# Local attention cut into ten windows of 64 keys, in place of nine windows of 72

## The chip, the cores and the metric

The kernel runs on one core of a Trainium2 chip, in one launch. The metric is the device time in microseconds (us) of that core, from one execution. The engines are TensorE (PE in the profile, with its weight loads as PEld), VectorE (DVE), ScalarE (ACT), GpSimd (POOL) and SyncE (SP), which issues nearly all of the DMAs.

## What is computed

Two kinds of attention on 2 batches of 8 heads of 576 tokens with 64 dimensions, whose outputs are added; then two feed-forward layers on the 1152 tokens of width 512. The change touches only the local attention.

```python
q_d = q.reshape(B, H, S // 4, 4, D).mean(axis=3)      # the same for k_d, v_d
out_up = np.repeat(sm_attn(q_d, k_d, v_d), 4, axis=2)
mask = np.abs(pos[:, None] - pos[None, :]) < 4
scores = np.where(mask, scale * q @ k.T, -1e9)
out_local = softmax(scores) @ v
x = out_up + out_local                                # heads side by side: 1152 x 512
h = x @ w_in;  g = np.where(h > 0, h, exp(min(h, 0)) - 1);  x = g @ w_out
# then four experts: sum_e p_e * relu(x @ w1[e]) @ w2[e], with 1024 hidden columns each
```

A query sees itself and three tokens on each side, so a chunk of n queries needs n + 6 keys.

## The kernel before

Heads are taken in pairs, eight pairs in all (`PAIRS`); a pair's two heads sit in partitions 0 to 63 and 64 to 127. The pairs 0 to 3 (batch 0) are worked on one after the other at the head of the kernel (mode ALONE, some 40 us). The pairs 4 to 7 (batch 1) are spread over the four blocks of the first feed-forward layer of batch 0 (mode MIXED): one pair to a block of 16 groups of matmuls (`mixed_block1`, L576). After that nothing of the attention is left, and the rest of the first layer and the four experts follow. The matmuls of the feed-forward layers are done in three products of a high and a low part (`product` L521, `product2` L593).

One pair takes these steps. `turn_q` and `turn_k` (L402, L411) bring q and k to 64 x 576 per head by transposes on TensorE. `score` (L425) has three parts j: j = 0 is the pooled attention, j = 1 and 2 are the local one, in chunks 0 to 3 and 4 to 8 of 64 queries (`SPANS` L39), each against a window of 72 keys (`WIN`). For the local parts a bf16 matmul of an identity and a band of 0 and -1e9 first writes the mask into the PSUM bank (L449), then the scores are added to it (L456). Both heads have matmuls of their own: head 0 on rows and columns 0 to 63 of the array, head 1 on rows and columns 64 to 127. Then DVE takes the row maxima of a part (`row_max` L1210), ACT the exponentials with their sums, chunk by chunk (`exponentiate` L867, line L877), DVE the reciprocals (L1221), and POOL multiplies (`normalise` L1620, line L1623). `turn_attn` (L461) transposes each chunk of 128 x 72 on its own; the last chunk, 8, has a place of its own in PSUM (`last_at` L99, line L487), the others four to a bank (L491). ACT copies them to SBUF (`copy_attnT` L882, lines L886 and L889). `mix` (L495) multiplies with v: first the pooled part (L510), then chunk by chunk and head by head (L516), 72 keys deep, head 0 into columns 0 to 63 and head 1 into columns 64 to 127. ACT copies the pooled result (L895), DVE adds both (`add_outputs` L1238, line L1246), and the sum is split into a high part (ACT L901) and a low one (DVE L1253).

In the trace an f32 matmul stands as two records of PE (two passes), each with its weight load; a transpose and the bf16 or fp32r matmuls are one record each.

All orders are written out by hand, engine by engine: for PE L780 to L848, for ACT L1089 to L1150, for POOL L1701 to L1728. In a mixed block (L576) the scores stand behind group 3, the three `turn_attn` behind groups 8, 10 and 11, and `mix` behind group 13. A group g waits until the bank of group g - 4 is free (`bank_free1` L529), which for g from 4 to 11 means that DVE has written its low part (`elu_lo` L1263, line L1266). ACT has the exponentials of the three parts in groups 4, 6 and 8, and the copies in 10 and 12 (L1135).

`load_v` (L320) loads the windows of v by four DMAs for a pair: for each head one with chunks 1 to 7 (L326) and one with chunks 0 and 8 (L329). SP issues, in this order, q of pair 0, q and k of pair 1, v of 0, q and k of 2, v of 1, q and k of 3, v of 2 and 3, q and k of 4, and only then the first weights `wa_raw` (L361) and `wb_raw` (L362). ACT turns the first weights into their high part (`first_wa` L1084, line L1087) at a fixed place in its order, between steps of pairs 1 to 3 (L1117).

## Time and profile before

| what | value |
|---|---|
| median of 3 runs | 647.47 us (647.23 to 647.62) |
| profiled execution, its own time | 647.4 us |
| its span in the trace | 645.6 us |
| PE busy | 638.2 us (99%), 4743 records |
| DVE, ACT, POOL busy | 349.4, 285.8, 323.2 us |
| granted TensorE clock | full over the whole span |
| DMA | 46.13 MB, mean 71 GB/s |

The busy time of an engine is the time in which at least one of its instructions is under way. A matmul of 64 columns stands in the trace with some 220 ns from its start to its end, and several are under way at once, so that the share of 99% says that PE seldom waits long; how dense the matmuls stand is read from their starts.

### The profile page before, as it was taken

To read this page: it belongs to the slowest core of one execution; us is meant where nothing else is said; L and a number is where in the kernel's file an instruction comes from. 1 tells how busy PE (TensorE), PEld (TensorE's weight loads), DVE (VectorE), ACT (ScalarE), POOL (GpSimd) and SP (SyncE) were. 2 spreads that over 40 slices of the span, in tenths; PEclk is the share of its full clock that TensorE was granted. 3 is DMA by queue.
4 is the path that set the end of the run, shared out by engine and by line. 5 is a ranking of instruction groups with operands and counts; after the bars stand their busy time and mean duration, and the time that the engine had idled before them with its cause. 6 is when DMAs were issued, how large, how long until landed. Compare 5 with 4: busy or idle time off the path is not lost.

```text
span 645.6 us, 13042 instructions
## 1 busy us (share of the span) xinstructions
PE 638.2 (99%) x4743; PEld 592.7 (92%) x4743; DVE 349.4 (54%) x764; ACT 285.8 (44%) x778; POOL 323.2 (50%) x278
## 2 busy tenths in 40 slices
PE   8999999999999999999999999999999999999998
PEld 5889999999999999998899899899899899889986
DVE  5976454545557787764453464355365255365352
ACT  4887474747476676553142152052152142142210
POOL 3684435353397999888238047056065164160200
PEclk9999999999999999999999999999999999999999
DMA  9963615142123223203003011011011012020012
GB/s 191 213 185 92 142 67 141 65 105 65 66 71 126 65 66 117 79 0 132 1 22 111 1 56 74 0 65 65 0 65 65 0 65 65 1 66 2 0 50 97
DMA packets 51491, 46.13 MB, mean 71 GB/s; under 512 B 31616, under 2 KB 33920, under 8 KB 51456
## 3 DMA queue, kind: packets, MB, share of 16 engines
q1 hardware_dynamic: 50272, 45.38, 23.9%
q10 hardware_dynamic: 1184, 0.30, 0.2%
q8 instruction: 21, 0.34, 0.2%
q14 instruction: 14, 0.11, 0.1%
HBM read 43.30 MB, written 2.36 MB: 71 GB/s over the span
## 4 chain that ended last, share of the span: by engine, by line
PE 94%; DVE 2%; ACT 1%; DMA 1%; issue 1%; POOL 0%; SPq 0%; DVEq 0%
PE psum L524 16%; PE psum L526 16%; PE psum L525 16%; PE psum L596 11%; PE psum L600 11%; PE psum L598 11%; PE psum L666 2%; PE psum L665 2%; PE psum L664 2%; PE psum L456 1%; PE psum L442 1%; PE psum L516 1%; PE psum L491 1%; PE psum L471 1%; DMA q_in<-in_q 1%; PE psum L570 1%
## 5 line engine op out<-in xcount | busy, mean ns | idle before, releaser
L1628 POOL TENSOR_TENSOR wb_lo<-wb_raw,wb_hi 128x512 fp32r<-128x512 f32 x64 | 81.8, 1298 | 183.3 <-ACT wb_hi L911 183.3
L1438 DVE SCALAR_TENSOR_TENSOR o_acc<-psum,gate_now,o_acc 128x512 f32<-128x512 f32 x72 | 54.0, 750 | 126.0 <-PE psum L526 125.7
L526 PE MATMUL psum<-wb_hi,h_lo 128*128 128x512 f32 x288 | 112.3, 390 | 0.0
L525 PE MATMUL psum<-wb_lo,h_hi 128*128 128x512 f32 x288 | 112.2, 390 | 0.0
L524 PE MATMUL psum<-wb_hi,h_hi 128*128 128x512 f32 x288 | 112.0, 389 | 0.0
L1021 ACT ACTIVATE h_hi<-psum 128x320 fp32r<-128x320 f32 (+1 forms) x128 | 52.5, 412 | 87.3 <-DVE psum L1410 40.3
L1628 POOL TENSOR_TENSOR wa_lo<-wa_raw,wa_hi 128x512 fp32r<-128x512 f32 x60 | 77.6, 1318 | 16.8 <-ACT wa_hi L952 16.8
L1027 ACT COPY sums<-psum 128x256 f32<-128x256 f32 (+1 forms) x32 | 12.8, 400 | 155.1 <-PE psum L600 155.1
L600 PE MATMUL psum<-x_hi,wa_lo 128*128 128x256 f32 (+2 forms) x228 | 67.4, 296 | 0.0
L598 PE MATMUL psum<-x_lo,wa_hi 128*128 128x256 f32 (+2 forms) x228 | 67.3, 295 | 0.0
L596 PE MATMUL psum<-x_hi,wa_hi 128*128 128x256 f32 (+2 forms) x228 | 67.2, 295 | 0.0
L526 PEld LDWEIGHTS psum<-wb_hi,h_lo 128*128 128x128 f32 x288 | 54.1, 188 | 11.3
L1392 DVE SCALAR_TENSOR_TENSOR h_lo<-psum,h_hi 128x320 fp32r<-128x320 f32 (+1 forms) x128 | 54.8, 450 | 17.1 <-ACT h_hi L1021 17.0
L525 PEld LDWEIGHTS psum<-wb_lo,h_hi 128*128 128x128 f32 x288 | 54.1, 188 | 10.9
L524 PEld LDWEIGHTS psum<-wb_hi,h_hi 128*128 128x128 f32 x288 | 54.1, 188 | 10.8
L524 PE MATMUL psum<-h_hi,wb_hi 128*128 128x288 f32 x160 | 48.9, 306 | 0.0
L526 PE MATMUL psum<-h_hi,wb_lo 128*128 128x288 f32 x160 | 47.1, 294 | 0.0
L525 PE MATMUL psum<-h_lo,wb_hi 128*128 128x288 f32 x160 | 47.1, 294 | 0.0
L598 PE MATMUL psum<-t_lo,s_hi 128*128 128x320 f32 (+2 forms) x152 | 44.9, 295 | 0.0
L600 PE MATMUL psum<-t_hi,s_lo 128*128 128x320 f32 (+2 forms) x152 | 44.8, 295 | 0.0
L596 PE MATMUL psum<-t_hi,s_hi 128*128 128x320 f32 (+2 forms) x152 | 44.8, 295 | 0.0
L596 PEld LDWEIGHTS psum<-x_hi,wa_hi 128*128 128x128 f32 x228 | 43.0, 189 | 0.6
(195 smaller groups left out, 1684.2 us busy)
## 6 DMA issues: line engine op xcount, KB each, us to landing
wa_raw<-in_moe_w_in SPq DMA_DIRECT2D x8, 1024.0 KB, 5.5
wb_raw<-in_moe_w_out SPq DMA_DIRECT2D x8, 1024.0 KB, 5.1
wa_raw<-in_moe_w SPq DMA_DIRECT2D x8, 1024.0 KB, 4.9
wb_raw<-in_moe_w SPq DMA_DIRECT2D x8, 1024.0 KB, 5.0
out<-o_acc SPq DMA_DIRECT2D x9, 256.0 KB, 2.0
q_in<-in_q SPq DMA_DIRECT2D x10, 144.0 KB, 3.9
v_in<-in_v SPq DMA_DIRECT2D x5, 288.0 KB
v_win<-in_v SPq DMA_DIRECT2D x10, 126.0 KB
```

Of the source, the lines that this page charges most:

```text
L524: nc.tensor.matmul(bank_cols, w_hi(n), x_hi_(n), start=(n == 0), stop=False)
L525: nc.tensor.matmul(bank_cols, w_hi(n), x_lo_(n), start=False, stop=False)
L526: last = nc.tensor.matmul(bank_cols, w_lo(n), x_hi_(n), start=False, stop=(n == chunks - 1))
L596: nc.tensor.matmul(bank, w_op[0][:, k, :], x_op[0][:, k, :], start=(start and k == 0), stop=False, skip_group_check=True)
L598: nc.tensor.matmul(bank, w_op[0][:, k, :], x_op[1][:, k, :], start=False, stop=False, skip_group_check=True)
L600: last = nc.tensor.matmul(bank, w_op[1][:, k, :], x_op[0][:, k, :], start=False, stop=(stop and k == 1), skip_group_check=True)
L664: nc.tensor.matmul(to, wb_hi[:, f, cols], h_hi[:, f, t], start=(f == 0), stop=False)
L665: nc.tensor.matmul(to, wb_hi[:, f, cols], h_lo[:, f, t], start=False, stop=False)
L1021: nc.scalar.activation(h_hi[:, 2 * fh + p, t0 + width * th:t0 + width * (th + 1)], psum[:, bank[p], 0:width], ACT.Relu).then_inc(h_hi_read ...
L1392: nc.vector.scalar_tensor_tensor(h_lo[at], bank(banks, p), 0.0, h_hi[at].bitcast(F32), ALU.max, ALU.subtract).then_inc(h_lo_ready, 1)
L1438: nc.vector.scalar_tensor_tensor(o_acc[:, m, :], psum[:, DOWN2_BANKS[(MT * half + m) % 2], :], gate_now[:, m:m + 1], o_acc[:, m, :], ALU.m ...
L1628: nc.gpsimd.tensor_tensor(lo[:, c, :], raw[:, c, :], hi[:, c, :].bitcast(F32), ALU.subtract).then_inc(lo_ready, 1)
```

## The change

The local attention is cut into ten chunks (slots) of at most 58 queries with windows of 64 keys, in place of nine of 64 queries and 72 keys. Even slots are the first half of the tokens and odd slots the second half (`TOK_AT`). A slot's scores are still computed for 64 queries (`Q_AT`), and only its own 58 (56 in the last two) are used by `mix`.

Slots 0 to 3 are part j = 1, slots 4 to 9 part j = 2. In part 2 the heads change places: head 0 writes to PSUM partitions 64 to 127 and head 1 to 0 to 63 (`part_of`). In the mixed blocks `local_scores` writes both masks and then issues the scores of the two parts by turns, so that four neighbouring matmuls lie in the four 64 x 64 corners of the array, and the two parts in two banks. In mode ALONE the parts stay apart.

`turn_attn` turns two slots (128 x 128) by one transpose, five in place of nine, with an even slot's keys in partitions 0 to 63 and an odd slot's in 64 to 127. The last chunk's own place, its waits and its copy are gone: `copy_attnT` makes two copies (128 x 256 and 128 x 384) in place of three. `v_win` has the windows of the even slots in partitions 0 to 63 and those of the odd slots in 64 to 127; it is loaded by eight DMAs in place of four. `mix` has 20 matmuls, 64 keys deep with 58 moving columns, in place of 18 of 72 keys with 64 columns, and goes round the four corners; the even slots' results go to one bank and the odd slots' to the other, in place of chunks 0 to 3 and 4 to 8. The exponentials are ten of 64 columns in place of nine of 72. In the lines left out, `OUT_SPLIT` becomes 288, the buffers and `band_of` follow the new shapes, `mixed_block1` calls `local_scores(u)` in place of parts 1 and 2 of `score`, PE's wait for `attnT_copied` ahead of `turn_q(3)` goes, and `copy_attnT_p` counts three transpose signals to a pair.

```diff
@@ -27,9 +27,14 @@
-NQT = SEQ // QT
-WIN = QT + 2 * FACTOR
-WIN_START = [min(max(QT * c - FACTOR, 0), SEQ - WIN) for c in range(NQT)]
+WIN = 64
+QSTEP = WIN - 2 * (FACTOR - 1)
+CHUNKS = -(-HALF // QSTEP)
+NQT = 2 * CHUNKS
+TOK_AT = [HALF * (s % 2) + QSTEP * (s // 2) for s in range(NQT)]
+TOK_N = [min(QSTEP, HALF - QSTEP * (s // 2)) for s in range(NQT)]
+Q_AT = [min(t, SEQ - QT) for t in TOK_AT]
+WIN_AT = [min(max(t - FACTOR + 1, 0), SEQ - WIN) for t in TOK_AT]
...
@@ -37,9 +42,8 @@
-LAST = NQT - 1
-BAND_RUNS = (None, ((0, 1), (1, 4)), ((4, LAST), (LAST, NQT)))
-BAND_PAD = QT * LAST - WIN_START[LAST]
+BAND_RUNS = (None, ((0, 1), (1, 4)), ((4, NQT - 1), (NQT - 1, NQT)))
+BAND_PAD = FACTOR - 1
...
@@ -96,11 +100,9 @@
-def last_at(u, mode):
-    if mode == MIXED:
-        return 0, 0
-    return (1, HALF) if u == HALF_PAIRS - 1 else (7, HALF)
+def part_of(h, j):
+    return slice(QT * h, QT * (h + 1)) if j < 2 else slice(QT * (1 - h), QT * (2 - h))
...
@@ -156,10 +158,10 @@
-                    spare[0:WIN, win_at:win_at + NQT * 2 * HD].rearrange("p (c h d) -> p c h d", h=2, d=HD))
+                    spare[:, win_at:win_at + CHUNKS * 2 * HD].rearrange("p (c h d) -> p c h d", h=2, d=HD))
         own_set = (sb1("q_in", [LT, NLT, 2 * HD])[:], sb1("k_in", [LT, NLT, 2 * HD])[:],
-                   sb1("v_in", [PT, 4, FACTOR * HD])[:], sb1("v_win", [WIN, NQT, 2, HD])[:])
+                   sb1("v_in", [PT, 4, FACTOR * HD])[:], sb1("v_win", [2 * WIN, CHUNKS, 2, HD])[:])
...
@@ -320,15 +322,17 @@
-                for h in range(2):
-                    at = rows.offset + h * SEQ * HD
-                    sp.dma_start(win[:, 1:NQT - 1, h, :],
-                                 bass.AP(rows.tensor, at + WIN_START[1] * HD,
-                                         [[HD, WIN], [QT * HD, NQT - 2], [1, HD]])).then_inc(win_loaded[held(u)], 16)
-                    sp.dma_start(win[:, 0:NQT:NQT - 1, h, :],
-                                 bass.AP(rows.tensor, at,
-                                         [[HD, WIN], [WIN_START[-1] * HD, 2], [1, HD]])).then_inc(win_loaded[held(u)], 16)
+                for e, (i0, odd) in enumerate(((1, 0), (0, CHUNKS - 1))):
+                    part = slice(WIN * e, WIN * (e + 1))
+                    for h in range(2):
+                        at = rows.offset + h * SEQ * HD
+                        sp.dma_start(win[part, i0:i0 + CHUNKS - 1, h, :],
+                                     bass.AP(rows.tensor, at + WIN_AT[2 * i0 + e] * HD,
+                                             [[HD, WIN], [QSTEP * HD, CHUNKS - 1], [1, HD]])).then_inc(win_loaded[held(u)], 16)
+                        sp.dma_start(win[part, odd, h, :],
+                                     bass.AP(rows.tensor, at + WIN_AT[2 * odd + e] * HD, [[HD, WIN], [1, HD]])
+                                     ).then_inc(win_loaded[held(u)], 16)
...
@@ -422,6 +426,27 @@
+            def band_masks(j, bank):
+                c0 = SPANS[j][0]
+                for n, (e0, e1) in enumerate(BAND_RUNS[j]):
+                    for h in range(2):
+                        rows = slice(HD * h, HD * (h + 1))
+                        nc.tensor.matmul(psum[part_of(h, j), bank, WIN * (e0 - c0):WIN * (e1 - c0)],
+                                         ident2[rows, rows], band_of(h, e0, e1), start=(n == 0), stop=False,
+                                         skip_group_check=True)
+            def local_score(u, j, s, bank):
+                at = WIN * (s - SPANS[j][0])
+                for h in range(2):
+                    rows = slice(HD * h, HD * (h + 1))
+                    last = nc.tensor.matmul(psum[part_of(h, j), bank, at:at + WIN],
+                                            qT[slot(u)][rows, Q_AT[s]:Q_AT[s] + QT], kT[slot(u)][rows, WIN_AT[s]:WIN_AT[s] + WIN],
+                                            start=False, stop=(s == SPANS[j][1] - 1), skip_group_check=True)
+                if s == SPANS[j][1] - 1:
+                    last.then_inc(scored, 1)
...
@@ -441,22 +466,22 @@
+                    last.then_inc(scored, 1)
                 else:
-                    c0, c1 = SPANS[j]
-                    for n, (e0, e1) in enumerate(BAND_RUNS[j]):
-                        for h in range(2):
-                            rows = slice(HD * h, HD * (h + 1))
-                            nc.tensor.matmul(psum[QT * h:QT * (h + 1), bank, WIN * (e0 - c0):WIN * (e1 - c0)],
-                                             ident2[rows, rows], band_of(h, e0, e1), start=(n == 0), stop=False,
-                                             skip_group_check=True)
-                    for c in range(c0, c1):
-                        s = WIN_START[c]
-                        for h in range(2):
-                            rows = slice(HD * h, HD * (h + 1))
-                            last = nc.tensor.matmul(psum[QT * h:QT * (h + 1), bank, WIN * (c - c0):WIN * (c - c0 + 1)],
-                                                    qT[slot(u)][rows, QT * c:QT * (c + 1)], kT[slot(u)][rows, s:s + WIN],
-                                                    start=False, stop=(c == c1 - 1), skip_group_check=True)
-                last.then_inc(scored, 1)
+                    band_masks(j, bank)
+                    for s in range(*SPANS[j]):
+                        local_score(u, j, s, bank)
+            def local_scores(u):
+                banks = [score_bank(u, j, MIXED) for j in range(3)]
+                band_masks(1, banks[1])
+                band_masks(2, banks[2])
+                first, second = range(*SPANS[1]), range(*SPANS[2])
+                for n in range(len(second)):
+                    if n < len(first):
+                        local_score(u, 1, first[n], banks[1])
+                    local_score(u, 2, second[n], banks[2])
...
@@ -474,22 +499,10 @@
-                if j == 2:
-                    if mode == MIXED:
-                        pe.wait_ge(attnT_p_copied, 2 * u + 1)
-                    elif u < 2:
-                        pe.wait_ge(qT_copied, u + 3)
-                    elif u == 2:
-                        pe.wait_ge(out_free, 2 * u + OUT_CREDIT)
-                    else:
-                        pe.wait_ge(qT_copied, HALF_PAIRS + 1)
-                    bank, at = last_at(u, mode)
-                    nc.tensor.transpose(psum[0:WIN, bank, at:at + 128], attn[:, LAST, :], ident[:]
-                                        ).then_inc(attn_turned, 1)
-                c0, c1 = SPANS[j]
-                for c in range(c0, min(c1, LAST)):
-                    last = nc.tensor.transpose(psum[0:WIN, TURN_BANKS[mode][j], 128 * (c - c0):128 * (c - c0 + 1)],
-                                               attn[:, c, :], ident[:])
+                for i in range(SPANS[j][0] // 2, SPANS[j][1] // 2):
+                    at = 128 * (i - SPANS[j][0] // 2)
+                    last = nc.tensor.transpose(psum[:, TURN_BANKS[mode][j], at:at + 128],
+                                               attn[:, 2 * i:2 * i + 2, :].rearrange("p e k -> p (e k)"), ident[:])
...
@@ -500,22 +513,23 @@
-                pe.wait_ge(win_loaded[held(u)], 64 * loads(u))
+                pe.wait_ge(win_loaded[held(u)], 128 * loads(u))
                 pe.wait_ge(attnT_p_copied, 2 * u + 2)
-                pe.wait_ge(attnT_copied, 3 * u + 3)
+                pe.wait_ge(attnT_copied, 2 * u + 2)
                 for kc in range(2):
                     for h in range(2):
                         nc.tensor.matmul(psum[HD * h:HD * (h + 1), banks[0], OUT_SPLIT:OUT_SPLIT + POOLED],
                                          v_sum[slot(u)][:, 2 * h + kc, :], attnT_p[slot(u)][:, kc, h, :], start=(kc == 0), stop=(kc == 1))
-                for half in range(2):
-                    c0, c1 = SPANS[half + 1]
-                    for c in range(c0, c1):
-                        for h in range(2):
-                            last = nc.tensor.matmul(psum[HD * h:HD * (h + 1), banks[half], QT * (c - c0):QT * (c - c0 + 1)],
-                                                    v_win[held(u)][:, c, h, :], attnT[:, c, QT * h:QT * (h + 1)],
-                                                    start=True, stop=True)
+                for i in range(CHUNKS):
+                    for e, h in ((0, 0), (1, 1), (0, 1), (1, 0)):
+                        c = 2 * i + e
+                        rows = slice(WIN * e, WIN * (e + 1))
+                        q0 = part_of(h, 1 if c < SPANS[1][1] else 2).start + TOK_AT[c] - Q_AT[c]
+                        last = nc.tensor.matmul(psum[HD * h:HD * (h + 1), banks[e], QSTEP * i:QSTEP * i + TOK_N[c]],
+                                                v_win[held(u)][rows, i, h, :], attnT[rows, i, q0:q0 + TOK_N[c]],
+                                                start=True, stop=True)
...
@@ -869,7 +881,7 @@
-                    act.wait_ge(attn_turned, 4 * (u - 1) + (1, 2, 4)[j])
+                    act.wait_ge(attn_turned, 3 * (u - 1) + j + 1)
...
@@ -880,14 +892,9 @@
-                if j == 2:
-                    act.wait_ge(attn_turned, 4 * u + 3)
-                    bank, at = last_at(u, mode)
-                    nc.scalar.copy(attnT[:, LAST, :], psum[0:WIN, bank, at:at + 128]).then_inc(attnT_copied, 1)
-                c0, c1 = SPANS[j][0], min(SPANS[j][1], LAST)
-                act.wait_ge(attn_turned, 4 * u + 2 * j)
-                nc.scalar.copy(attnT[:, c0:c1, :], psum[0:WIN, TURN_BANKS[mode][j], 0:128 * (c1 - c0)]
-                               ).then_inc(attnT_copied, 1)
+                i0, i1 = SPANS[j][0] // 2, SPANS[j][1] // 2
+                act.wait_ge(attn_turned, 3 * u + j + 1)
+                nc.scalar.copy(attnT[:, i0:i1, :], psum[:, TURN_BANKS[mode][j], 0:128 * (i1 - i0)]).then_inc(attnT_copied, 1)
...
```

## Rows read from the trace of the kernel before

**Rows 1.** The page: busy us, share of the span, and instructions of each engine.

```profile
PE 638.2 (99%) x4743; PEld 592.7 (92%) x4743; DVE 349.4 (54%) x764; ACT 285.8 (44%) x778; POOL 323.2 (50%) x278
```

**Rows 2.** Busy us by stretch: length, PE, PEld, DVE, ACT, POOL, clock, DMA share, GB/s.

```profile
5.00:40.30 35.30, 32.68 (x533) 27.82 (x533) 29.26 (x69) 28.93 (x123) 21.91 (x27) 1.00 0.94 213
...
46.00:167.00 121.00, 121.00 (x1202) 118.46 (x1202) 63.35 (x160) 73.58 (x239) 56.96 (x53) 1.00 0.37 100
...
22.00:34.00 12.00, 11.45 (x203) 9.74 (x203) 11.77 (x28) 10.29 (x49) 10.64 (x15) 1.00 0.97 246
```

**Rows 3.** Groups by line and shape, PE: busy us, mean ns of one | idle.

```profile
L491 PE MATMUL psum<-ident,attn 128*72 128x128 f32 x64 | 9.6, 273 | 0.0
...
L516 PE MATMUL psum<-attnT,v_win 72*64 72x64 f32 x180 | 6.1, 222 | 0.0
```

**Rows 4.** Timeline of PE, scores of the second mixed block: start us, us from first start to last end.

```profile
78.88 0.95 PE L442 MATMUL psum<-kTs,qTs 64*64 64x144 f32 x12
79.67 0.29 PE L449 MATMUL psum<-band,ident 64*64 64x72 bf16 x4
79.80 0.67 PE L456 MATMUL psum<-kT,qT 64*64 64x72 f32 x16
80.30 0.32 PE L449 MATMUL psum<-band,ident 64*64 64x288 bf16 x4
80.45 0.82 PE L456 MATMUL psum<-kT,qT 64*64 64x72 f32 x20
81.20 0.40 PE L524 MATMUL psum<-x_hi,wa_hi 128*128 128x288 f32 x1
```

**Rows 5.** Timeline of PE, two narrow windows at the first two records of L442.

```profile
46.12 0.33 PE L442 MATMUL psum<-kTs,qTs 64*64 64x144 f32 x1
...
46.12 0.34 PE L442 MATMUL psum<-kTs,qTs 64*64 64x144 f32 x2
```

**Rows 6.** Timeline of PE, the mix of the second mixed block.

```profile
99.66 1.22 PE L516 MATMUL psum<-attnT,v_win 72*64 72x64 f32 x36
100.81 0.41 PE L524 MATMUL psum<-h_hi,wb_hi 128*128 128x288 f32 x1
```

**Rows 7.** Timelines of DVE, ACT and PE around group 8 of two mixed blocks.

```profile
87.28 0.43 DVE L1266 TENSOR_TENSOR h_lo<-psum,h_hi 128x288 fp32r<-128x288 f32 x1
...
87.77 0.40 PE L524 MATMUL psum<-h_hi,wb_hi 128*128 128x288 f32 x1
...
49.55 1.28 DVE L1218 TENSOR_SCALAR neg_max<-neg_max 128x3 f32<-128x3 f32 x1
...
51.13 0.36 ACT L877 ACTIVATE attn_p<-psum,neg_max 128x144 f32<-128x144 f32 x1
```

**Rows 8.** Groups by line and shape, ACT: the local exponentials and the copies.

```profile
L877 ACT ACTIVATE attn<-psum,neg_max 128x72 f32<-128x72 f32 x72 | 22.0, 327 | 0.2 <-PE psum L491 0.2
...
L889 ACT COPY attnT<-psum 72x512 f32<-72x512 f32 x16 | 9.4, 586 | 6.8 <-PE psum L491 6.8
...
L886 ACT COPY attnT<-psum 72x128 f32<-72x128 f32 x8 | 2.1, 265 | 0.3
```

**Rows 9.** Timelines of DVE and PE in the head, with the idle time before.

```profile
22.03 0.53 DVE L1224 TENSOR_SCALAR sums<-sums 128x3 f32<-128x3 f32 x1 [0.70 <-ACT attn_p L877]
...
34.56 0.17 DVE L1224 TENSOR_SCALAR sums<-sums 128x5 f32<-128x5 f32 x1 [0.43 <-ACT attn L877]
...
37.66 0.37 PE L570 MATMUL psum<-x_hi,wa_hi 128*128 128x288 f32 x1 [0.47 <-DVE x_sum L1246]
```

**Rows 10.** SP: issues of L329 (ns min/median/max), first weights (us to landing), ACT's use.

```profile
L329 SPq DMA_DIRECT2D v_win<-in_v x10: 305/408/2964, 6.0 to 135.7; - x10
...
wa_raw<-in_moe_w_in SPq DMA_DIRECT2D x1, 1024.0 KB, 6.7
...
27.23 0.51 SPq L361 DMA_DIRECT2D wa_raw<-in_moe_w_in  x1
...
34.98 0.63 ACT L1087 CAST wa_hi<-wa_raw 128x512 fp32r<-128x512 f32 x1
```

More of the change, by code:

```diff
@@ L84 @@
 BANK_A, BANK_B, BANK_C = (0, 3), (1, 4), (2, 5)
-OUT_SPLIT = QT * SPANS[1][1]
+OUT_SPLIT = HALF
 OPEN = (4, 2)
@@ L175, in program @@
         attn_p = sb1("attn_p", [128, NPQ, POOLED])
-        attnT = sb1("attnT", [WIN, NQT, 128])
+        attnT = sb1("attnT", [2 * WIN, CHUNKS, 128])
         attnT_p = (sb1("attnT_p", [PT, 2, 2, POOLED])[:],
@@ L225, in band_of @@
         def band_of(h, c0, c1):
-            at = BAND_PAD + QT * h - (QT * c0 - WIN_START[c0])
+            at = BAND_PAD + QT * h - (Q_AT[c0] - WIN_AT[c0])
             run = band[HD * h:HD * (h + 1), at:at + WIN]
@@ L1228, in copy_attnT_p @@
             def copy_attnT_p(u, mode):
-                dve.wait_ge(attn_turned, 4 * u + 1)
+                dve.wait_ge(attn_turned, 3 * u + 1)
                 if mode == ALONE and u >= 2:
```

4 lines of the change are left out of this document (1 added, 3 removed).

## The prediction

> **What bounds the kernel.** I read the page first [rows 1]: PE is busy for 638.2 of 645.6 us. That alone could still hide loose matmuls, so the next view is the busy time by stretch [rows 2]. In the mixed blocks, from 46 to 167 us, PE is busy for 121.00 of 121.00 us while DVE and ACT work 63 and 74 us: what is taken off PE there should come off the time, unless one step of DVE or ACT stands exactly where PE needs it. In the head, from 5 to 40.3 us, it is another matter: PE is busy 32.7 of 35.3 us, but DVE and ACT are close behind, and from 22 to 34 us DVE is busy for 11.77 of 12.00 us. There three engines take turns at being the bound. Then I read the starts of the matmuls in the timeline, since a matmul stands with 222 ns [rows 3] however short it is.
>
> **How dense the small matmuls stand.** In the mix [rows 6] 36 records take 1.22 us from the first start to the last end. Less the last one's 0.222 that is 1.00 us; if the records go in 18 pairs there are 17 steps of 58.7 ns for 64 columns. The same sum for 20 records of the scores [rows 4], (0.82 - 0.222) / 9, gives 66 ns, and for 16 records (0.67 - 0.222) / 7 = 64 ns, for 72 columns: about 0.8 ns for each column more. The transposes go one by one: 64 of them in 16 groups are busy 9.6 us [rows 3], 0.60 us to a group; (0.60 - 0.273) / 3 = 109 ns for 128 columns, 0.85 ns a column. So one f32 record costs 0.85 ns a column in its own corner, and two corners work side by side. The narrow windows [rows 5] show it directly: two records of L442 end only 0.01 us later than one, so the second starts 10 ns or less behind the first.
>
> **The change, part by part** (for one pair of heads).
>
> Transposes. Nine become five, all of 128 moving columns; the deeper and wider operand costs nothing that a row shows, since the step is set by the moving columns. Saved: 4 x 0.109 = 0.44 us.
>
> Mix. 40 records in place of 36, of 58 columns: a step is 58.7 - 6 x 0.8 = 53.9 ns. If all four corners work side by side, 40 records are 10 steps, 0.54 us. Going from the 72-deep pooled matmuls to 64-deep ones is a new change of the array's shape. The nearest row: from the last start of L516, at 99.66 + 17 x 0.0587 = 100.66, it is 0.15 us to L524 at 100.81, 0.09 more than a step [rows 6]. Bounds nothing and 0.09; I take 0.07. Before 18 x 0.0587 = 1.06 us, after 0.61: saved 0.45 us.
>
> Scores in a mixed block. Before, from the first mask to the next group, 79.67 to 81.20 [rows 4]: 1.53 us. After, part 2 is the longer chain: its masks have 320 + 64 columns; the masks of 360 columns took 80.30 to 80.45, 0.42 ns a column, so 0.16 us; then 6 slots x 2 passes = 12 steps of 58.7 ns, 0.70 us. Part 1 (8 steps) runs in the two other corners beside it, but its masks are issued ahead, 0.04 us, and the way out costs 0.09. Sum 0.99: saved 0.54 us. In the head the parts stay apart: 8 + 12 steps of 58.7 ns for 8 + 10 of 65, 1.17 for 1.17 us, nothing.
>
> ACT. The copies: 265 ns for 128 columns and 586 for 512 [rows 8] are 0.84 ns a column, so 256 and 384 columns take 0.37 and 0.48: 0.85 for 1.44 us. One exponential more costs 22.0 / 72 = 0.31 us, and nine are 8 columns shorter (7 ns each): in all 0.3 us less for ACT. The row maxima of DVE and the product of POOL read 640 in place of 648 columns: nothing.
>
> The exponential more lies in part 2. In a mixed block it makes the third part's weights ready some 0.25 us later, while PE gets to the third `turn_attn` sooner. I cost that at nothing because ACT has 47 us to spare in 121 [rows 2]; if that cover were gone it would be 0.25 us a block, 1 us in all.
>
> DMAs. Four more for a pair, of the same bytes within 2%. In the mixed blocks SP is idle. In the head 16 more are issued ahead of the first weights. The least time of an issue is 305 ns [rows 10]. But the DMA engines are nearly full there (share 0.94 to 0.97 [rows 2]), so the bytes set the pace and the issues wait for them. The weights are issued at 27.23 and land 6.7 us later, at 33.9; ACT first uses them at 34.98: 1.05 us of cover, 0.7 once the head is shorter. I expect up to 0.7 us of delay and cost it at nothing. Without the cover every microsecond goes straight into ACT's order, with the copies behind it on which PE waits.
>
> **The sum.** Mixed blocks 1 to 3: 0.44 + 0.45 + 0.54 = 1.43 us each, 4.3 us. Does group 8 let it through? It starts at 87.77, and the low part it waits for ends at 87.28 + 0.43 = 87.71 [rows 7]: no slack. But that chain starts from PE's group 4, behind the scores, and moves with it. Block 0 is tighter: ACT's pooled exponentials (51.13) start only 0.3 us behind DVE's scaled maximum (49.55 + 1.28 = 50.83), a step of 1.28 us that was held up. PE arrives there some 1.3 us sooner, DVE perhaps not. I leave 0.35 of the 1.43 there: 1.1 us.
>
> The head. Its savings on PE would be 4 x (0.44 + 0.45) = 3.6 us at most. DVE is the chain from 22.03 to 34.56 [rows 9], and its work doesn't shrink; it starts from ACT's exponentials ending at 22.03, and ahead of them ACT has its copies 0.59 us shorter and one more exponential, and PE four transposes less. So the chain moves by 0.35, and with it the DVE addition for which PE waits until 37.66. Behind that `mix` of pair 3 is on PE's own path: 0.45 more. Head 0.8 us, bounds nothing and 3.6.
>
> 4.3 + 1.1 + 0.8 = 6.2 us off. The profiled execution took 647.4 us, the median of the runs is 647.47: both give 641.3 us.
>
> **The rivals.**
> (a) Only two records go side by side. No row shows more than two corners at work. Then the mix has 20 steps of 53.9 ns and 0.07, 1.15 for 1.06 us; the scores have 20 of 58.7 ns, 640 mask columns at 0.42 ns and the way out, 1.53 for 1.53; only the transposes gain: 0.35 us a block. Four blocks and 0.3 in the head are 1.7 us: 645.7. A mechanism would be strict order: the program issues both passes of one head's matmul and then both of the other's; if a pass could not go by one that waits for its corner, each matmul would cost one full step whatever corners its neighbours use. Against it: six matmuls of 144 columns, 12 records, take 0.95 us [rows 4]. In strict order there would be seven starting times at least 144 x 0.83 = 0.12 us apart and 0.33 for the last, 1.05 us. So a pass does go by at least one other. For it: how far it may go by is not shown.
> The Trainium skill, page "TensorE: Matmul & The Clock Gate", Part 3, "The mechanism", has that rule: matmuls are "strict FIFO, no reordering". By that rule the time would be that of (a); the 0.95 us speak against it. Chance of (a) 0.16.
> (b) DVE and ACT hold the mixed blocks. Group 8 has no slack, so if its chain did not move with group 4 the 0.54 us of the scores would be lost four times: 2.2 us, 643.5. Against it: ACT and DVE are idle for about two fifths or more of these blocks [rows 2]. Chance 0.12.
> (c) Slower: the first weights come late. If SP's issues and not the bytes set the pace, 16 more at the median of 408 ns [rows 10] are 6.5 us: the weights land at 40.4, ACT stands still for 5.8 us with every step of pairs 2 and 3 behind it, and the gain is eaten up but for some 0.4 us. At 0.7 us for each issue, as a held-up queue gives, it is 11.2 us, 10.5 of them beyond the cover: 647.4 - 6.2 + 10.5 = 651.7. It decides from 0.51 us an issue on, where the delay beyond the cover is 7.5 us. Against it: the DMA share of 0.94. Chance 0.04.
>
> **How the numbers follow.** Forecast 0.66, (a) 0.16, (b) 0.12, (c) 0.04, anything else 0.02. The forecast's own range is 640.0 to 642.6: the head from 0.3 to 2 us, the way between shapes, block 0. To hold 8 in 10 it has to take in (b) and half-way cases of (a) (three corners at once, or four for part of the rounds): 639.8 to 645.0. Below lies only a head that gives back more than 2 us. What a measurement can tell is 0.2%, 1.3 us. Forecast, (a) and (b) all end more than that below 647.47, (a) by little: faster 0.92, same 0.04, slower 0.04.
>
> **What would show it.** In a mixed block: five transposes in two groups of PE's timeline, 109 ns apart; 40 records of the mix within some 0.75 us (0.47 and one's length); the scores from first mask to next group in about 1.0 us. Three records starting within some 20 ns of the first would show more than two corners. The way from the scores of one block to those of the next, 46.12 to 78.88 [rows 5, 4] or 32.8 us, would be 31.0 to 31.4. The first weights' use by ACT near 34.6, with little idle time on a DMA. The forecast is wrong if the mix still takes 1.2 us (then (a)), if idle time of PE appears ahead of group 8 or of `turn_attn` (then (b)), or if ACT stands idle before the first weights (then (c)).

## The result, and the profile after

The changed kernel is **slower** by 0.9%, which is clear of the noise: 653.29 us median of 6 runs (652.08 to 653.80) against 647.53 us (647.23 to 647.74) of the kernel before on the same chip, a ratio of 1.0086 (95% interval 1.0073 to 1.0099). The forecast was 641.3 us; the third rival, (c), the late first weights, had 651.7. The profiled execution took 653.07 us, with a span of 651.3.

The first view is again the page.

```profile
PE 635.3 (98%) x4775; PEld 587.2 (90%) x4775; DVE 348.7 (54%) x764; ACT 283.2 (43%) x786; POOL 321.7 (49%) x278
PEclk9789999999999999999999999999999999999999
PE 91%; SPq 5%; DMA 1%; ACT 1%; issue 1%; DVE 0%; DVEq 0%
```

Two things are new beside [rows 1]. PE has 2.9 us less to do and the span is 5.7 us longer, so the time was lost in waiting. And in the third row, the shares of the chain of work that ended last, SP's queue holds 5% of the span, 30 us or so: the engine that only issues transfers has become a bound.

Where, the starting times of the mixed blocks tell. The timeline of PE, at the zeros matmul that opens the scores of each:

```profile
56.77 0.19 PE L463 MATMUL psum<-zeros 128*128 128x64 bf16 x1
...
88.58 0.21 PE L463 MATMUL psum<-zeros 128*128 128x64 bf16 x1
...
119.92 0.21 PE L463 MATMUL psum<-zeros 128*128 128x64 bf16 x1
...
151.25 0.21 PE L463 MATMUL psum<-zeros 128*128 128x64 bf16 x1
```

The kernel before has this matmul at 46.00, 78.75, 111.47 and 144.18 us. So the distances are 31.81, 31.34 and 31.33 us where they were 32.75, 32.72 and 32.71: block 0 gains 0.94 us and blocks 1 and 2 gain 1.4 each. The whole loss is ahead of the first: 56.77 against 46.00, 10.8 us.

Inside a mixed block, the scores and the mix of the changed kernel in the timeline of PE:

```profile
88.72 0.83 PE L467 MATMUL psum<-kTs,qTs 64*64 64x144 f32 x10
89.27 0.32 PE L435 MATMUL psum<-band,ident 64*64 64x320 bf16 x2
89.38 0.29 PE L467 MATMUL psum<-kTs,qTs 64*64 64x144 f32 x2
...
89.62 0.81 PE L444 MATMUL psum<-kT,qT 64*64 64x64 f32 x38
90.36 0.40 PE L538 MATMUL psum<-x_hi,wa_hi 128*128 128x288 f32 x1
...
108.52 0.81 PE L530 MATMUL psum<-attnT,v_win 64*64 64x58 f32 x40
109.26 0.40 PE L538 MATMUL psum<-h_hi,wb_hi 128*128 128x288 f32 x1
```

From the zeros matmul to the next group the scores take 1.78 us (88.58 to 90.36), where they took 2.45 (78.75 to 81.20, [rows 4] has the end). The mix takes 0.74 us from its first start to the next group, where it took 1.15 [rows 6]: 40 records in less time than 36.

Now the head. The busy time by stretch (length, PE, PEld, DVE, ACT, POOL, granted clock, DMA share, GB/s):

```profile
10.00:15.00 5.00, 4.43 (x65) 3.67 (x65) 4.71 (x12) 4.62 (x27) 3.17 (x5) 1.00 0.73 156
15.00:20.00 5.00, 4.83 (x81) 3.94 (x79) 4.83 (x13) 4.24 (x22) 2.14 (x3) 1.00 0.41 97
20.00:25.00 5.00, 2.01 (x55) 1.58 (x52) 2.83 (x11) 2.48 (x16) 3.27 (x5) 0.85 0.65 144
25.00:30.00 5.00, 4.77 (x55) 3.96 (x55) 2.00 (x4) 2.36 (x10) 2.25 (x4) 0.50 0.52 117
```

The DMA share was 0.94 over the head of the kernel before, from 5 to 40.3 us [rows 2]; here it is 0.67 over the same stretch and falls to 0.41 in one part of it. The DMA engines have room, and nobody gives them work. The timeline of SP shows why:

```profile
5.22 0.74 SPq L330 DMA_DIRECT2D v_win<-in_v  x1
6.00 0.60 SPq L333 DMA_DIRECT2D v_win<-in_v  x1
6.65 0.62 SPq L330 DMA_DIRECT2D v_win<-in_v  x1
7.31 0.62 SPq L333 DMA_DIRECT2D v_win<-in_v  x1
...
38.22 0.51 SPq L365 DMA_DIRECT2D wa_raw<-in_moe_w_in  x1
```

Each window transfer costs 0.62 us of SP's time, and the next begins 0.04 us later: SP is seldom held up (four issues of the head take over 1 us); the issues themselves are long. That goes on for 32 of them, and the first weights are issued at 38.22 in place of 27.23 [rows 10]. Over all loads of these two lines (ns min/median/max):

```profile
L330 SPq DMA_DIRECT2D v_win<-in_v x20: 621/625/741, 5.2 to 145.8; - x20
L333 SPq DMA_DIRECT2D v_win<-in_v x20: 472/563/631, 6.0 to 146.6; - x20
```

The last of them are in the mixed blocks, where SP's queue is idle: no congestion makes them long. The old ones had a least time of 305 ns [rows 10].

Who waited for it, in timelines of ACT and PE and in the waits of PE (us in total, times, longest):

```profile
45.02 0.62 ACT L1094 CAST wa_hi<-wa_raw 128x512 fp32r<-128x512 f32 x1 [5.17 <-DMA wa_raw<-in_moe_w_in]
47.08 0.58 PE L584 MATMUL psum<-x_hi,wa_hi 128*128 128x288 f32 x1 [3.45 <-DVE x_sum L1253]
```

```profile
PE psum L584 <- DVE x_sum L1253: 3.5, 1, 3.5
PE psum L411 <- DMA h_spare<-in_q: 3.0, 1, 3.0
PE psum L419 <- DMA k_in<-in_k: 2.1, 1, 2.1
```

The queries of pair 3 arrive late (3.0 us of PE), then the keys of pair 4 (2.1 us); ACT stands idle for 5.17 us before the weights. It uses them at 45.02 in place of 34.98, 10.0 us later. PE opens its groups at 47.08 in place of 37.66 [rows 9], 9.4 later, and the last 1.35 us come behind that: behind PE's waits the granted clock is 0.50, the lower of the two levels, until 50.84 us, and the stretch to the first mixed block takes 9.69 us (47.08 to 56.77) in place of 8.34. PE has no idle time in either stretch.

### The profile page after: what moved, and what is told of

It is laid out like the page before. It is cut to its first block, busy times and chain, and to the rows that moved or that the text cites. A ratio compares the mean times of both kernels' runs of the same rounds, so it can differ in the third digit from the quotient of the medians.

```text
span 651.3 us, 13151 instructions
## 1 busy us (share of the span) xinstructions
PE 635.3 (98%) x4775; PEld 587.2 (90%) x4775; DVE 348.7 (54%) x764; ACT 283.2 (43%) x786; POOL 321.7 (49%) x278
## 4 chain that ended last, share of the span: by engine, by line
PE 91%; SPq 5%; DMA 1%; ACT 1%; issue 1%; DVE 0%; DVEq 0%
PE psum L538 16%; PE psum L540 16%; PE psum L539 16%; PE psum L609 11%; PE psum L613 11%; PE psum L611 11%; PE psum L679 2%; PE psum L678 2%; PE psum L677 2%; SPq L330 2%; SPq L333 2%; DMA wa_raw<-in_moe_w_in 1%; SPq L312 1%; SPq L316 1%; PE psum L530 1%
## 5 line engine op out<-in xcount | busy, mean ns | idle before, releaser
L1028 ACT ACTIVATE h_hi<-psum 128x320 fp32r<-128x320 f32 (+1 forms) x128 | 52.4, 411 | 87.4 <-DVE psum L1417 40.3
L538 PEld LDWEIGHTS psum<-wb_hi,h_hi 128*128 128x128 f32 x288 | 54.1, 188 | 10.8
```

The source lines that it names most:

```text
L538: nc.tensor.matmul(bank_cols, w_hi(n), x_hi_(n), start=(n == 0), stop=False)
L1028: nc.scalar.activation(h_hi[:, 2 * fh + p, t0 + width * th:t0 + width * (th + 1)], psum[:, bank[p], 0:width], ACT.Relu).then_inc(h_hi_read ...
```

## The experiments

Theory **S**, formed on these rows: it is the shape of a transfer that costs, not the count; one of exactly 64 partitions keeps SP about twice as long. The rivals: the count of transfers does it (**N**), or something in their order or bytes. Each ratio below is to the kernel before on the same chip (medians of 647.46 to 647.72 us); a difference between two experiments is one of medians, of which some come from two chips.

**1. The kernel before with twice as many window transfers.** Its four per pair of heads become eight, all still 72 partitions.

```diff
-                    sp.dma_start(win[:, 1:NQT - 1, h, :], ...)
-                    sp.dma_start(win[:, 0:NQT:NQT - 1, h, :], ...)
+                    for c0, c1 in ((1, 5), (5, 8), (0, 1), (8, 9)):
+                        sp.dma_start(win[:, c0:c1, h, :], ...)
```

> The kernel before, with its four window DMAs of v for a pair cut into eight (chunks 1 to 4, 5 to 7, 0 and 8 for each head), still 72 partitions each; nothing else. Theory N (the number of issues counts, whatever their shape): with 0.6 us for each issue as in the changed kernel, four more for each of four pairs put the first weights some 7 to 9 us later than in the kernel before, and the time is 653 to 656 us. Theory S (the shape counts, 64 partitions of a window against 72): an issue of 72 partitions stays at 0.31 to 0.45 us, the DMA engines stay the bound, the first weights move by less than 2 us and the time stays within 1.5 us of 647.5.

Measured: 648.91 us (10 runs, 647.23 to 652.25), ratio 1.0023 (1.0005 to 1.0042), +1.35 us. The issues of the head mostly took 0.37 to 0.42 us, and the first weights left at 30.29 us, 3.1 later than in the kernel before where S allowed 2; the profiled execution (650.03 us) is one of the longer ones. The count costs something, but a quarter of the loss.

**2. The change with its windows at an even step.** Its windows at the two ends break the step of 58, and so need transfers of their own. With the second half's windows moved to 280 + 58i, four transfers of 64 partitions bring a pair.

```diff
-WIN_AT = [min(max(t - FACTOR + 1, 0), SEQ - WIN) for t in TOK_AT]
+WIN_AT = [QSTEP * (s // 2) + (s % 2) * (SEQ - WIN - QSTEP * (CHUNKS - 1)) for s in range(NQT)]
...
-                for e, (i0, odd) in enumerate(((1, 0), (0, CHUNKS - 1))):
+                for e in range(2):
+                    for h in range(2):
+                        sp.dma_start(win[WIN * e:WIN * (e + 1), :, h, :], ...)
```

> The changed kernel with windows at an even step of 58 in both halves of the tokens (first slot takes 61 queries, the last of the second half too), so that four window DMAs of 64 partitions x 5 windows stand for a pair in place of eight; the matmuls are as many and as wide, but for the widths of two slots in each half. Theory N and theory S both: four issues of 0.62 us in place of eight take 2.6 us less for a pair on SP; the first weights are issued 9 to 10 us sooner than at 38.2, near 28 to 29 us, PE's waits for q of pair 3 and for q and k of pair 4 go, and the time falls to 641 to 644 us, below the kernel before. Rival M (the gaps in the head come from the matmuls or from the lower clock, not from SP): the time stays near 653.

Measured: 643.03 us (642.58 to 645.31), ratio 0.9926 (0.9910 to 0.9943): **faster** than the kernel before, by 0.7%, with transfers of 64 partitions. The issues still took 0.62 us, now 16 of them in the head and not 32. In the profiled execution, the longest of the four at 645.31 us, the weights left at 30.15, later than the 28 to 29 expected, and this row of ACT's waits says what was left:

```profile
ACT wa_hi L1090 <- DMA wa_raw<-in_moe_w_in: 1.4, 1, 1.4
```

**3. The change with another order of SP.** The first weights go ahead of the v of pair 3, the later queries and keys ahead of the earlier v.

```diff
             load_q(0)
             load_qk(1)
-            load_v(0)
             load_qk(2)
-            load_v(1)
+            load_v(0)
             load_qk(3)
+            load_v(1)
             load_v(2)
-            load_v(3)
             qk_used(0)
             load_qk(HALF_PAIRS)
             sp.dma_start(wa_raw[:], w_in_v[0]).then_inc(wa_loaded, 16)
             sp.dma_start(wb_raw[:], w_out_v[0]).then_inc(wb_loaded, 16)
+            load_v(3)
```

> The changed kernel with its eight window DMAs, but in another order on SP: q and k of pair 2 ahead of v of pair 0, q and k of pair 3 ahead of v of pair 1, and v of pair 3 behind the first weights. The sum of SP's issues is the same. If the loss is that q, k and the first weights stand behind the window issues: no wait of PE for q of pair 3, first weights issued at 31 to 33 us in place of 38.2, so landed near 38 to 39, some 4 us late: 645 to 648 us. If the DMA engines' own time for the small pieces were the bound, the order would give back less than 2 us: above 651.

Measured: 655.11 us, ratio 1.0119 (1.0092 to 1.0145): worse than the change itself. The weights left at 31.72 and nobody waited for queries, but the wait only changed its place:

```profile
PE psum L504 <- POOL attn L1630: 11.9, 2, 10.9
```

POOL's `sum_v(3)` stands ahead of its `normalise(3, 1)` and needs the v of pair 3, now behind the weights; PE's transposes wait for POOL. The new wait is not one for SP's issues. SP issued that v at 32.82 us, and POOL could start on it at 44.00. The two first weights, 1 MB each, had been issued ahead of it at 31.72 and 32.27, and `wb_raw` landed at 42.55. The busy time by stretch shows full DMA engines meanwhile, and the granted clock falling while PE waits:

```profile
32.00:38.00 6.00, 3.19 (x63) 2.27 (x61) 3.43 (x11) 3.26 (x19) 0.32 (x1) 0.94 1.03 320
38.00:44.00 6.00, 0.00 (x0) 0.00 (x0) 0.82 (x2) 1.33 (x3) 0.00 (x1) 0.50 1.09 198
```

So this order took the wait for the queries away and put one behind the bytes of the weights in its place. Other orders were not tried.

**4. The length of an issue, by shape.** Behind the kernel's last store, with idle queues, each transfer alone and twice; the table has the shorter of the two.

> The kernel before, and behind its last store, with nothing else under way, 14 shapes of DMA from v to SBUF, each issued twice and waited for: 72 partitions with 7, 4, 2 and 1 pieces of 256 bytes, 64 with 7, 4, 2 and 1, and 4 pieces with 80, 96, 128, 32, 65 and 63 partitions. The time is longer by these DMAs, some 28 x 2.5 = 70 us, and tells nothing. Theory S: SP's issue takes 0.3 to 0.4 us for 72 partitions and 0.6 for 64; theory N: all take the same. What 63, 65, 96 and 128 take says whether it is the number of partitions or a single odd case.

Measured, SP's issue in ns, rows of 256 bytes:

| partitions x rows each | ns | | partitions x rows each | ns |
|---|---|---|---|---|
| 72 x 7 | 328 | | 64 x 7 | 601 |
| 72 x 4 | 300 | | 64 x 4 | 595 |
| 72 x 2 | 301 | | 64 x 2 | 596 |
| 72 x 1 | 308 | | 64 x 1 | 488 |
| 65 x 4 | 315 | | 63 x 4 | 273 |
| 80 x 4 | 336 | | 96 x 4 | 312 |
| 128 x 4 | 391 | | 32 x 4 | 328 |

One partition more or one less makes it about half as long.

**5 and 6. One partition moved.** The kernel before, each window transfer of 72 partitions cut into two: 63 + 9 in the one kernel, 64 + 8 in the other. Same count, same bytes. The edit of 64 + 8, shortened:

```diff
-                    sp.dma_start(win[:, 1:NQT - 1, h, :], ...)
-                    sp.dma_start(win[:, 0:NQT:NQT - 1, h, :], ...)
+                    for p0, p1 in ((0, 64), (64, WIN)):
+                        sp.dma_start(win[p0:p1, 1:NQT - 1, h, :], ...)
+                        sp.dma_start(win[p0:p1, 0:NQT:NQT - 1, h, :], ...)
```

> The kernel before with each window transfer of 72 partitions cut by its partitions into one of 63 and one of 9: 8 per pair of heads in place of 4, as many as in the change. Theory S: 0.27 to 0.36 us each, as in b_split, first weights issued at 29 to 30.5, time 648 to 649.5. Rival N (the count alone slows the change's head): 8 transfers cost it the change's loss, about +5 us over 647.5.

> The same cut one partition further on, 64 and 8: same count, same bytes, but half of the new transfers now span exactly 64 partitions. Theory S: those issue in 0.60 to 0.74 us against 0.27 to 0.36, 16 of them in the head, so the first weights are issued 16 x 0.3 = 4.8 us later than in b_63_9, at 34 to 35.5, and the time is 3 to 5 us over b_63_9. Rival N: no difference from b_63_9 beyond 0.5 us.

Measured: 63 + 9 took 648.32 us (10 runs, 647.43 to 654.22), ratio 1.0028 (1.0005 to 1.0052); 64 + 8 took 652.80 us (4 runs, 651.64 to 653.19), ratio 1.0073 (1.0058 to 1.0089). One partition moved, and the median is 4.5 us higher. The issues of L327, first 63 + 9, then 64 + 8:

```profile
L327 SPq DMA_DIRECT2D v_win<-in_v x20: 278/284/993, 5.2 to 142.0; - x20
```

```profile
L327 SPq DMA_DIRECT2D v_win<-in_v x20: 342/602/1018, 5.1 to 144.1; - x20
```

The expected place of the delay was wrong, though: the first weights were issued at 30.90 and 31.98 us, 1.1 us apart and not 4.8. The 32 window issues of the head add up to 16.7 us with 63 + 9, many of them held up, and to 16.4 with 64 + 8. But the profiled execution of 63 + 9 was one of its long ones (652.27 us, 4 above its median) and says little of how that kernel mostly runs. Six of its ten runs took 647.4 to 648.3 us with a mean granted clock of 1.00; the other four took 650.4 to 654.2 with 0.992 to 0.997. All four runs of 64 + 8 have 0.995 to 0.997. So a part of the 4.5 us is probably the lower clock that goes with a wait of PE (2.1 and 2.9 us in the two profiled executions), and not the issues alone. The verdict here rests on the medians and on the lengths of the issues, and number 7 is the cleaner test.

**7. The change, each transfer one row short.** The straightest test: uneven windows, eight transfers per pair, order and all else as in the change, but 63 partitions.

```diff
-                    part = slice(WIN * e, WIN * (e + 1))
+                    part = slice(WIN * e, WIN * (e + 1) - 1)
...
-                                             [[HD, WIN], [QSTEP * HD, CHUNKS - 1], [1, HD]])).then_inc(win_loaded[held(u)], 16)
+                                             [[HD, WIN - 1], [QSTEP * HD, CHUNKS - 1], [1, HD]])).then_inc(win_loaded[held(u)], 16)
...
-                        rows = slice(WIN * e, WIN * (e + 1))
+                        rows = slice(WIN * e, WIN * (e + 1) - 1)
```

> The change as it stands, its uneven windows and its 8 window transfers per pair of heads among it, but each transfer brings 63 of the 64 rows, and the mix reads 63 rows: the last key of every window is left out of the local mix, so the output differs from the reference by that key. Count and order of the transfers, scores, transposes and all other work are the change's. Theory S (the shape of exactly 64 partitions, not the count): issues of 0.27 to 0.40 us where the change has 0.56 to 0.62, first weights issued at 29 to 31 in place of 38.22, time 642.5 to 645. Rival N (eight transfers per pair are the loss, whatever their shape): weights after 35, time 650 to 653.

Measured: **642.20 us** (4 runs, 641.85 to 644.30), ratio 0.9926 (0.9900 to 0.9951). 11.1 us lower than the change, for 1 row in 64, and 0.3 below the range expected. In both, SP issues 54 transfers ahead of the first weights. The 32 window issues add up to 22.1 us in the change and to 13.4 here, and the weights left at 29.14.

```profile
L330 SPq DMA_DIRECT2D v_win<-in_v x20: 278/291/863, 5.1 to 132.9; - x20
L333 SPq DMA_DIRECT2D v_win<-in_v x20: 288/334/1671, 5.5 to 133.4; - x20
```

**8. A whole kernel without the shape.** Windows of 63 keys at an even step of 57 (60, 57, 57, 57, 57 tokens in the first half, mirrored in the second), in slots that stay 64 wide, their last column masked: the reference's computation in full, four transfers of 63 partitions to a pair.

```diff
-QSTEP = WIN - 2 * (FACTOR - 1)
-CHUNKS = -(-HALF // QSTEP)
+KEYS = 63
+QSTEP = KEYS - 2 * (FACTOR - 1)
+CHUNKS = (HALF - FACTOR + 1) // QSTEP
...
+                for e in range(2):
+                    for h in range(2):
+                        sp.dma_start(win[WIN * e:WIN * e + KEYS, :, h, :], ...)
```

> The windows of a_uniform made 63 keys wide, at an even step of 57, in slots that stay 64 wide; every one of the 16 window transfers of the head then spans 63 partitions and none 64. Nothing but one masking matmul of one column per head is added. Theory S (a transfer of exactly 64 partitions costs SP about twice the issue): the window issues in the head fall from 0.62 us (a_uniform) to 0.27 to 0.35, so SP reaches the first weights some 16 x 0.3 = 4.8 us ahead of a_uniform's 30.15, or where the bytes allow, at 25.5 to 27.5; ScalarE's wait of 1.38 us for the first weights goes, and the time falls from 643.0 to 640.5-642, the forecast that the change was given. Rival N (the count of transfers or their bytes set the pace, not their shape): issues in the head stay at 0.5 to 0.6, weights at 29.5 to 30.2, and the time within 0.5 of 643.0.

Measured: **642.40 us** (5 runs, 642.13 to 642.54), ratio 0.9918 (0.9905 to 0.9932), 5.1 us under the kernel before. The granted clock is 1.00 throughout, and ACT waits for no weights. The weights left at 29.30, later than the 25.5 to 27.5 expected: seven issues of this head took 1 to 2 us, and its 16 window issues add up to 9.9 us where number 2's made 11.2. The time is 0.4 us above what was expected of it, and only 0.6 below number 2. With 16 window transfers the shape matters little: the DMA share of number 2 was 1.02 from 5 to 38 us, so there the bytes were the bound again.

**9. The four corners undone.** Number 8, with the parts of the scores one behind the other and the mix first in the upper 64 partitions and then in the lower.

```diff
-                        local_scores(u)
+                        score(u, 1, MIXED)
+                        score(u, 2, MIXED)
...
-                for i in range(CHUNKS):
-                    for e, h in ((0, 0), (1, 1), (0, 1), (1, 0)):
+                for e in range(2):
+                    for i, h in [(i, h) for i in range(CHUNKS) for h in range(2)]:
```

> a_keys63 with the four corners undone and nothing else: the two parts of the local scores follow each other in the mixed blocks, and the mix takes all windows of the upper 64 partitions ahead of the lower, so that only two neighbouring corners have records side by side. Theory F (four corners work at once only where the program order brings them together): scores of a mixed block back from 1.76 to about 2.3 us from the zeros matmul to the next group, the mix's 40 records from 0.8 to about 1.2 us: +0.9 us per mixed block, +3 to +4.5 us over a_keys63 in all. Rival O (the array lets passes of an idle corner go ahead by itself, so the order hardly matters): within 0.6 us of a_keys63.

Measured: 646.03 us (10 runs, 645.61 to 646.22), ratio 0.9974 (0.9965 to 0.9983); 3.6 us over number 8. The mix, this kernel's row and then number 8's:

```profile
98.79 1.20 PE L532 MATMUL psum<-attnT,v_win 63*64 63x60 f32 x40
```

```profile
97.78 0.81 PE L532 MATMUL psum<-attnT,v_win 63*64 63x60 f32 x40
```

The same 40 records take 0.39 us longer, and from the zeros matmul to the next group it is 2.32 us (78.31 to 80.63) in place of 1.78. Together that is the 0.93 us by which blocks 1 and 2 grow; block 0 grows by 0.50, and the head, from its first scores to the first mixed block, by 0.38 (38.69 us for 38.31). So the order in the program decides: where ten or so matmuls stand between those of the one pair of corners and those of the other, the two pairs of corners did not work side by side.

**10. More shapes.** As number 4.

> The kernel before, with test transfers behind its last store on an idle queue, each waited for before the next, each twice; their time counts for nothing, only the length of SP's issue. Shapes: 64 partitions starting at partition 0, 32 and 64, 63 starting at 64, 64 and 63 with rows of 1024 bytes, 128, 112, 62, 60, 56, 48, 32, 16 and 8 partitions. Theory S in its narrow form (the count of exactly 64 partitions): only the 64s issue in 0.5 to 0.75 us, wherever they start and however long a row, all others in 0.27 to 0.40. Wider form (any count that fills a power of two or a multiple of 16 in some pattern): 16, 32 or 128 would stand out as well, or 64 would not with rows of 1024 bytes.

Measured, the shorter of two, in ns: 64 partitions x 4 rows from partition 0, 64 and 32: 596, 595, 591; with rows of 1024 bytes 613. 63 x 4 from partition 64: 301, with rows of 1024 bytes 280. 128 x 2: 390, 128 x 1: 346, 112 x 4: 317, 62 x 4: 234, 60 x 4: 329, 56 x 4: 316, 48 x 4: 312, 32 x 8: 327, 16 x 4: 312, 8 x 7: 278, 8 x 2: 272. Two rows of its timeline of SP, the second 64 and the second 63:

```profile
647.81 0.60 SPq L400 DMA_DIRECT2D wa_raw<-in_v  x1
...
656.28 0.30 SPq L400 DMA_DIRECT2D wa_raw<-in_v  x1
```

Only the 64s stand out, wherever they start and however long a row: S in its narrow form.

**11. Where the head's gain went.** Number 8 gains nothing until the first mixed block (46.05 us, before 46.00). Its added exponential is left out in the head for pairs 1 to 3.

```diff
-                for c in range(c0, c1):
+                for c in range(c0, c1 - 1 if mode == ALONE and u > 0 and j == 2 else c1):
```

> a_keys63 with the last exponential of part 2 left out in the head for pairs 1 to 3 (so each of them has nine local exponentials, as the kernel before; the tenth window keeps the weights and the sum of pair 0, and the output differs there). It asks where the head's forecast gain of 0.8 us went: a_keys63 starts its first mixed block at 46.05 us, the kernel before at 46.00. Theory E (the added exponential, 0.29 to 0.31 us, stands on the chain ScalarE - VectorE of the head, three times): first mixed block at 45.1 to 45.6 us, time 641.3 to 642.0. Rival V (VectorE's own work is the chain, and the exponential lies beside it, as ScalarE's idle 0.82 us before its last part suggests): first mixed block within 0.2 us of 46.05, time within 0.3 of 642.4.

Measured: 642.70 us (6 runs, 641.84 to 645.93), against number 8's 642.40. The median shows no gain, but the runs lie far apart (three at 641.84 to 642.02, three at 643.37 to 645.93), so the time can't decide. The profiled execution began later as a whole, so that only distances can be compared: from the zeros matmul of pair 1 to the first mixed block 32.37 us (14.78 to 47.15), in number 8 32.66 (13.39 to 46.05). Of three exponentials left out 0.3 us is found, one's worth, where E had 0.45 to 0.95. So the exponentials are at most a part of the missing gain.

## Why the prediction was wrong, and where it was right

**The step that failed: "DMAs ... cost it at nothing".** It said that "the bytes set the pace and the issues wait for them", from a DMA share of 0.94 and a least issue of 305 ns. That held for the transfers of the kernel before; the change made others. No row could show a transfer of 64 partitions: the kernel before has 72, 96 and 128. The step took the price of the nearest row, a least time of 0.31 us, for window transfers that cost about 0.62 us each. Number 7 puts the loss on that: one row less in each transfer gives 11.1 us, and the time lands at 642.2.

An estimate from these rows says when the price matters. SP issues almost without a break in the head, so the weights leave after the sum of the issues ahead of them, 0.75 us at the start and some 0.045 us between two: 24.8 us for 38 issues before, 35.1 for 54 in the change, 26.0 for 54 in number 7. SP's 22 issues other than the windows take 13.0 us in the change. With 32 window issues of 0.4 us, as in number 1, the weights would leave at 29 us (they left at 30.3 there), 2 later than before and with half of that covered. With 32 of 0.62 they leave at 36 even if nothing is held up. With number 2's 16 of 0.62 it would be 25.4, earlier than the bytes allow. So doubling the count alone costs little, a length of 0.62 us alone costs little, and both together make SP the bound.

**Rival (c) happened, and that its upper price is near is partly luck.** It priced 16 added issues at 0.408 or 0.7 us, the 0.7 for a queue held up by the bytes. Here that was about the length of an issue of its own, with nothing holding it up. The window issues of the head grew from 9.5 us for 16 (0.59 each, from 0.37 to 0.99, some of them held up by the bytes) to 22.1 for 32 (0.69 each), while SP's other 22 shrank from 15.3 to 13.0. That makes 10.3 of the 11.0 us by which the weights are late; 16 more gaps of 0.04 us are the rest. Its "decides from 0.51 us an issue on" is right in kind, and 651.7 is 1.6 below the time. What it left out: PE's waits for the queries of pair 3 and the keys of pair 4, and the lower clock behind them. Its chance of 0.04 was argued from the DMA share. That share says who was the bound; it says nothing of how near the next one is. SP spent 24.8 of its first 27.2 us issuing, held up or not, and a lengthening of each was the case to price.

**Mixed blocks: right.** 1.43 us a block were forecast and 1.4 measured for blocks 1 and 2, 1.1 for block 0 and 0.94 measured, with and without the trouble in the head (number 8: 0.96). By parts: the mix 0.41 (forecast 0.45), the scores 0.67 (0.54; from the first mask it is 1.09 us where 0.99 was forecast, but the first masks now start under the pooled scores), the transposes 0.22 in each of their two groups (0.60 to 0.38 us, and 0.71 to 0.49), 0.44 (0.44). The parts make 1.52; 0.12 is lost somewhere between the groups.

**Rival (a), two records side by side: wrong.** Had it been right, the mix's 40 records would take over 1.1 us and not 0.74, and number 9 would cost nothing over number 8. It costs 3.6 us. By the Trainium skill, page "TensorE: Matmul & The Clock Gate", Part 3, "The mechanism", matmuls are "strict FIFO, no reordering". This trace disagrees as far as records go: two masks (L435) start at 89.27 us, and two records of the pooled scores (L467), which the program issues ahead of them, at 89.38. These two are the last of twelve, so they can be the second passes of matmuls whose first passes started ahead of the masks; that a whole matmul was overtaken no row shows.

**Rival (b): not seen.** No wait of PE appears ahead of group 8 or of the transposes of a block. Why block 0 gains 0.45 us less than the others, of which the forecast had laid 0.35 to DVE, was not looked into.

**The head: 0.8 forecast, 0.2 at most found.** From the first pooled scores to the first mixed block number 8 takes 38.31 us (7.74 to 46.05) and the kernel before 38.49 (7.51 to 46.00). The forecast let ACT's shorter copies move the chain at 22.03 us by 0.35. Counted from the first scores the chain is there at the same time, 14.5 us on, in both (22.03 and 22.25): ACT now stands idle for DVE's row maxima three times, 1.6 us in all between 12 and 40 us, in number 8. So DVE was probably the bound before 22 us as well, where it was busy for 4.5 of each 5 us from 10 to 20 us before, and for 4.7 and 4.8 in number 8; that this explains all of the missing 0.6 us is argued and not shown.

With the head's 0.0, block 0's 0.96 and 1.4 for each of three, number 8 comes to 5.2 us, and 5.1 were measured. The forecast's 6.2 was too high by the head's 0.8 and some tenths. (Its sum is a tenth off as well: 6.2 from 647.4 is 641.2.)

## What to carry to other kernels

A change of tile shape changes its transfers too: price each new shape of transfer by a row of its own shape, and where there is none, keep a factor of two in hand on a queue that is busy without a break. An engine that only issues can be the next bound right behind full DMA engines; when the DMA share falls while the data come late, look at the issuing queue. Transfers of exactly 64 partitions are to be avoided where SP's queue is on the path: here 63 rows in place of 64 in each of the change's transfers made a loss of 0.9% into a gain of 0.7% (number 7). Half as many transfers did the same with 64 partitions (number 2), and both together gave 0.8% (number 8). Small matmuls in four corners paid here only where the program issues them by turns: undone, it cost 3.6 us.

## What the runs showed of the hardware

**64 partitions.** An issue from SP takes 0.59 to 0.61 us for 64 partitions and two or more rows, 0.27 to 0.33 for 63, 65 and 72, and 0.39 for 128, in one and the same trace; a single row of 64 partitions takes 0.49. It holds from partitions 0, 32 and 64, for rows of 256 and of 1024 bytes. Why, no run here shows.

**A short issue is not a short transfer.** 62 partitions have the shortest issue of the larger ones, 0.23 us, but each of its two tests kept the queue 3.1 us or more until the next, where 60 and 63 partitions needed 1.7 to 1.9. By the Trainium skill, page "DMA: Bandwidth & Descriptors", section "Why a DMA increments its semaphore by 16 and not by 1", a transfer runs on the largest number of engines up to 16 that divides its outermost sizes. That makes 2 engines for 62 partitions, 9 for 63 and 15 for 60. The times agree with it.

**The clock as a second loss.** In the changed kernel PE waited 3.0 us for queries, until 24.57 us, and the granted clock was 0.85 from 20 to 25 us and 0.50 from 25 to 30; then it waited 2.1 us until 42.61 and 3.5 us until 47.08, and the clock was 0.90 from 40 to 45 us and 0.50 from 45 to 50. In number 8, where the longest wait of PE in the head after its start is 1.24 us, it was 1.00 in every stretch of the head.
